# One program block for attention, its general path and the expert layers; the first tokens prepared inside the last pair of heads; alpha transposed behind all of y

## The reference

```python
# attention: q, k, v, alpha are (4, 8, 768, 48), alpha in 0.8 to 1.0
for t in range(S):
    state = alpha[:, :, t, :, None] * state + k[:, :, t] (x) v[:, :, t]
    y[:, :, t] = q[:, :, t] @ state
x = y as 3072 tokens x 384                      # transpose and reshape
# first layer, d_ff 2048
h = x @ w_in
g = (a0 + a1*h + a2*h^2 + a3*h^3) / (1 + |b0||h| + |b1|h^2 + 1e-6)
x2 = g @ w_out
# second layer, d_ff 1024
h = x2 @ w_in2;  solu = h * softmax(h)
out = layernorm(solu) * g_ln @ w_out2
```

## Time and profile before

| | us |
|---|---|
| median of 3 runs | 836.74 (834.29 to 837.64) |
| profiled execution, its own time | 835.56 |
| span of its instructions | 833.8 |
| busy: PE, PEld | 787.8, 733.2 |
| busy: DVE, ACT, POOL | 689.5, 606.4, 313.1 |
| mean granted TensorE clock | 0.987 |

### The profile page before, as it was taken

How to read it: one execution, slowest core, us unless ns; L and a number is a source line. 1 busy time by engine, 2 the same in 40 slices (tenths; PEclk the granted TensorE clock), 3 DMA queues, 4 the chain that set the end, 5 groups by cost and what they waited for, 6 DMA issues and landing times.

```text
span 833.8 us, 16287 instructions
## 1 busy us (share of the span) xinstructions
PE 787.8 (94%) x5378; PEld 733.2 (88%) x5378; DVE 689.5 (83%) x1248; ACT 606.4 (73%) x1258; POOL 313.1 (38%) x376
## 2 busy tenths in 40 slices
PE   5989999869889999999999999999999999999986
PEld 4777777769879999999999999999999999999975
DVE  5888888669999888988889888898889888898642
ACT  5777788568878776887678867787778777687522
POOL 5999886412223222332223323232333322233201
PEclk8999999999999999999999999999999999999998
DMA  8999997410000010001000100000000000000000
GB/s 178 223 233 234 241 206 180 110 44 1 19 11 1 11 39 1 11 11 39 9 1 9 38 9 0 12 36 9 9 28 9 9 9 9 1 11 10 11 9 29
DMA packets 113174, 42.96 MB, mean 52 GB/s; under 512 B 101616, under 2 KB 110960, under 8 KB 113136
## 3 DMA queue, kind: packets, MB, share of 16 engines
q1 hardware_dynamic: 110336, 33.04, 16.8%
q0 software_dynamic: 2800, 9.45, 3.9%
HBM read 33.04 MB, written 9.44 MB: 51 GB/s over the span
## 4 chain that ended last, share of the span: by engine, by line
PE 61%; DVE 10%; ACT 6%; issue 2%; DVEq 0%; POOL 0%; ACTq 0%
PE h_ps L919 17%; PE acc_ps L945 17%; PE y_ps L901 13%; PE z_ps L964 12%; DVE work L1160 2%; PE z_ps L974 2%; DVE rec L1152 2%; DVE den L1148 2%; ACT rec L1054 1%; ACT g_hi L1044 1%; DVE den L1165 1%; ACT rec L1056 1%; DVE solu L1124 1%; DVE work L1168 1%; ACT den L1019 1%
## 5 line engine op out<-in xcount | busy, mean ns | idle before, releaser
L1102 POOL TENSOR_TENSOR g_lo<-work,g_hi 128x384 fp32r<-128x384 f32 x128 | 130.8, 1022 | 406.0 <-ACT g_hi L1044 406.0
L919 PE MATMUL h_ps<-x,w 128*128 (+1 forms) x1152 | 227.8, 342 | 9.8 <-DVE work L1170 4.6
L945 PE MATMUL acc_ps<-g_hi,w 128*128 128x384 f32 x768 | 218.4, 338 | 2.2 <-POOL g_lo L1102 2.2
L919 PEld LDWEIGHTS h_ps<-x,w 128*128 128x128 f32 x1152 | 203.5, 189 | 16.0 <-DVE work L1170 8.8
L945 PEld LDWEIGHTS acc_ps<-g_hi,w 128*128 128x128 f32 x768 | 141.2, 188 | 2.8 <-POOL g_lo L1102 2.8
L1016 ACT ACTIVATE h<-h_ps 128x384 f32<-128x384 f32 x128 | 61.7, 482 | 101.9 <-PE h_ps L919 101.9
L945 PE MATMUL acc_ps<-g_lo,w 128*128 128x384 f32 x384 | 129.6, 338 | 0.0
L901 PE MATMUL y_ps<-w,lnT 128*128 128x384 f32 x576 | 111.8, 344 | 2.7 <-DVE ysb L1191 2.7
L1165 DVE SCALAR_TENSOR_TENSOR den<-h,ncoef,den 128x384 f32<-128x384 f32 x128 | 78.6, 614 | 42.5 <-ACT den L1019 41.5
L901 PEld LDWEIGHTS y_ps<-w,lnT 128*128 128x128 f32 x576 | 104.8, 193 | 4.9 <-DVE lnT L1182 3.0
L964 PE MATMUL z_ps<-w,x 128*128 128x512 f32 x414 | 104.3, 397 | 3.3 <-DVE lnT L1182 3.3
(11 more groups left out here) (116 smaller groups left out, 1140.8 us busy)
## 6 DMA issues: line engine op xcount, KB each, us to landing
work<-in_alpha_dram SPq DMA_DIRECT2D x32, 144.0 KB, 3.4
chunks_xin<-in_q_dram SPq DMA_DIRECT2D x32, 144.0 KB, 3.2
chunks_xin<-in_k_dram SPq DMA_DIRECT2D x32, 144.0 KB, 3.1
chunks_vin<-in_v_dram SPq DMA_DIRECT2D x16, 288.0 KB, 4.0
wstage<-in_moe_w_in_dram POOLq DMA_DIRECT2D x9, 512.0 KB, 4.8
attention_out<-solu SPq DMA_DIRECT2D x32, 144.0 KB, 3.1
out_dram<-ysb SPq DMA_DIRECT2D x24, 192.0 KB, 1.8
x<-attention_out SPq DMA_DIRECT2D x7, 576.0 KB, 3.9
```

The costliest lines, as they stand in the source:

```text
L919: mm = nc.tensor.matmul(h_ps[s % 2][:, 0:TT], w1[:, wz, kc, s * P:(s + 1) * P], xs[:, xz, kc, :], start=(n == 0), stop=(n == 3 * KC - 1))
L945: mm = nc.tensor.matmul(acc_ps[:, dc, 0:TT], w2[:, wz, f, dc * P:(dc + 1) * P], rhs, start=(f == 0 and n == 0), stop=(f == FC1 - 1 and n = ...
L1102: nc.gpsimd.tensor_tensor(g_lo[:, 1 - o, :], gate[:, 1 - o, :], g_hi[:, 1 - o, :].bitcast(F32), ALU.subtract).then_inc(glo_done, 1)
```

## The change

It has four parts.

1. The three blocks become one. `attention_by_chunks` and `attention_by_scan` now return their programs for each engine, and these are called at the head of the layers' block. The barriers go. In their place the four engines with a branch wait for a semaphore `judged`, which comes with `fits`; POOL, PE and DVE then raise `joined`, and every engine waits for `joined` = 3 and for all 32 y copies before its part of the layers.
2. In body 16 (the last pair's stage 2) ACT makes the high part of the first tokens at the head of the body, DVE the low part ahead of its first mask, and PE the first chunk of h between turning kp back and the products of chunks 4 and 5. It waits there for all weight pieces. For this the tile `x` takes the place of tiles that are dead by then, and `h_ps` is the tile that was `turn_aq`. The general path makes the three again from its own results.
3. The transposes of alpha stand behind `before` of chunks 3 to 5, in every body.
4. In body 16 the counting matmul stands ahead of that last `before`.

```diff
+def first_h(nc, over):
+    KC, TT = over.x.shape[3:]
+    for kc in range(KC):
+        for n, (wz, xz) in enumerate(PARTS):
+            mm = nc.tensor.matmul(over.h_ps[:, 0, 0:TT], over.w1[:, wz, kc, 0:P], over.x[:, 0, xz, kc, :],
+                                  start=(kc == 0 and n == 0), stop=(kc == KC - 1 and n == 2))
+    return mm
...
 # attention_by_chunks, tensor, body
                         mm.then_inc(kt_turned, 1)
+            if i_is(n, NPAIR):
+                pe.wait_ge(w_lo, over.w_pieces)
+                pe.wait_ge(over.x_ready, over.x.shape[3])
+                first_h(nc, over).then_inc(over.h_ready, 1)
...
                         for c in range(CPH + 1, NC):
                             within(p, c)
+                if i_is(n, NPAIR):
+                    pe.wait_ge(tally, 6)
+                    nc.tensor.matmul(ring[0:1, 0, 0:1], okay[:, 4:5], ones[:], start=True, stop=True).then_inc(counted, 1)
+                for c in range(CPH, NC):
+                    mm = before(p, c)
+                mm.then_inc(y_done, 1)
                     if stage1(n + 1):
                         pe.wait_ge(a_loaded[1 - o], (i + o + 1) * 32)
                         pe.wait_ge(rec_done, n + 1)
                         turn(ain[:, 1 - o], turn_aq, a_turned, CPH)
-                    if stage2(n):
-                        for c in range(CPH, NC):
-                            mm = before(p, c)
-                        mm.then_inc(y_done, 1)
...
 # scalar, body
+            if i_is(n, NPAIR):
+                act.wait_ge(x0_loaded, 16)
+                act.wait_ge(k_turned, NPAIR)
+                act.wait_ge(ksq_seen, NPAIR)
+                for kc in range(over.x.shape[3]):
+                    nc.scalar.activation(over.x[:, 0, HI, kc, :], x0_of(over.work, *over.x.shape[3:])[:, kc, :],
+                                         ACT.Copy).then_inc(over.xhi_done, 1)
...
 # vector, body
+            if i_is(n, NPAIR):
+                dve.wait_ge(kp_ready, NPAIR)
+                for kc in range(over.x.shape[3]):
+                    dve.wait_ge(over.xhi_done, kc + 1)
+                    nc.vector.tensor_tensor(over.x[:, 0, LO, kc, :], x0_of(over.work, *over.x.shape[3:])[:, kc, :],
+                                            over.x[:, 0, HI, kc, :].bitcast(F32), ALU.subtract).then_inc(over.x_ready, 1)
...
 # attention_by_scan, tensor (gpsimd, sync and vector alike)
-            @block.tensor
-            def _(pe):
+    def tensor(pe):
+        pe.wait_ge(judged, 1)
                 with pe.If(pe.value_load(fits, min_val=0, max_val=1) != 1):
...
+        pe.sem_inc(joined, 1)
...
 # the layers' block
+        def attention_over(eng):
+            eng.wait_ge(joined, 3)
+            eng.wait_ge(att_copied, NB * NH)
...
             def _(pe):
+                chunks.tensor(pe)
+                scan.tensor(pe)
+                attention_over(pe)
...
-                        if g is not None:
+                        if g is not None and not (i_is(i, 0) and s == 0):
...
             def _(act):
+                chunks.scalar(act)
+                attention_over(act)
...
-                for kc in range(KC):
-                    x_hi(0, kc)
...
-                for kc in range(KC):
-                    x_lo(0, kc)
```

More of the change, by code:

```diff
@@ L39 @@
 PARTS = ((HI, HI), (HI, LO), (LO, HI))
+@dataclass
+class Programs:
+    sync: object
+    gpsimd: object
+    tensor: object
+    scalar: object
+    vector: object
+@dataclass
+class Handover:
+    work: object
+    x: object
+    w1: object
+    h_ps: object
+    att_stored: object
+    x0_loaded: object
+    xhi_done: object
+    x_ready: object
+    h_ready: object
+    y_copied: object
+    judged: object
+    w_pieces: int
 def wait_alone(eng, semaphore, value, carrier):
@@ L172, in halves @@
             return t.rearrange("p (z t) -> p z t", z=2)
[L174 to L246, removed]
-            @block.tensor
-            def _(pe):
[L250 to L255, removed]
-                def attention_products(p, chunks):
-                    for c in chunks:
-                        for j in range(2):
-                            rows = slice(j * HB, j * HB + D)
-                            mm = nc.tensor.matmul(ring[:, j, (c % 4) * P:(c % 4 + 1) * P], kp[rows, c * P:(c + 1) * P],
-                                                  qp[rows, p, c * P:(c + 1) * P], start=True, stop=True)
-                    mm.then_inc(att_done, 1)
-                def within(p, c):
@@ L478, in attention_by_scan @@
+    return Programs(sync, gpsimd, tensor, scalar, vector)
+def attention_by_scan(nc, ctx, q, k, v, alpha, scratch, ident, fits, w_lo, neg_done, solu, over):
     NB, NH, S, D = q.shape
@@ new lines, in gpsimd @@
+    def gpsimd(pool):
+        pool.wait_ge(judged, 1)
+        with pool.If(pool.value_load(fits, min_val=0, max_val=1) != 1):
+            pool.wait_ge(y_copied, NB * NH)
+            nc.gpsimd.memset(xin[:], 0.0).then_inc(zeroed, 1)
+            nc.gpsimd.memset(blockones[:], 0.0).then_inc(zeroed, 1)
+            pool.wait_ge(zeroed, 2)
+            for j in range(2):
+                nc.gpsimd.memset(blockones[j * HB:(j + 1) * HB, j * HB:(j + 1) * HB], 1.0).then_inc(zeroed, 1)
+                pool.wait_ge(zeroed, 3 + j)
+            nc.gpsimd.tensor_tensor(onehot[:], ident[:, 0:HB], ident[:, HB:P], ALU.add).then_inc(zeroed, 1)
+            pool.wait_ge(zeroed, 5)
+        pool.wait_ge(w_lo, over.w_pieces)
+        pool.wait_ge(neg_done, 1)
+        pool.sem_inc(joined, 1)
@@ L658, in build @@
         solu = sb("solu", [P, F2])
+        h_ps = ps("h_ps", [P, 2, 512])
+        with ExitStack() as guests:
+            homes = [sb("chunks_" + name, shape, F32, guests) for name, shape in
+                     (("xin", [P, 2, S // P, HB + D]), ("rec", [P, S]), ("err", [P, S]), ("att", [P, 2, S // P, P]), ("causal", [P, P]), ("okay", [P, 5]))]
+        x = sb("x", [P, 2, 2, KC, TT], F32R)
         phase_a = ExitStack()
```

723 lines of the change are left out of this document (401 added, 322 removed).

## The result

| | before | changed |
|---|---|---|
| median, us | 837.19 (834.29 to 837.96, 4 runs) | 827.08 (825.71 to 828.42, 4 runs) |
| profiled execution, its span | 835.56, 833.8 | 826.95, 825.2 |
| mean granted clock | 0.987 | 0.996 |

The ratio is 0.9885 (95%: 0.9856 to 0.9915): 10 us faster, where 827.5 was forecast. Two later sets of runs of the same kernel gave 0.9919 (0.9889 to 0.9949) and 0.9883 (0.9857 to 0.9909), so the gain is 7 to 10 us.

The account below looks back on a forecast made before the run. It took a ring of waits among ACT, DVE and TensorE to bound the attention, and the layers' start to bound the rest. 3.9 + 4.7 + 0.7 - 0.3 = 9.0 us gave 827.5 us, range 824 to 831.

Parts of the forecast that it names:

- last `kp` to first square, clock apart: From the last pair to the layers: ACT's first h at K+12.85 instead of K+17.53, 4.7 us gained (K: last `kp` start).
- second h late: In the layers: the second chunk's h, due in 2.73 us, takes 3.3 at the lower clock; 0.3 us charged.
- the ring through ACT's copy, `err` and `rec`: In each attention pair: ACT, DVE and TensorE wait on one another in turn, said to set the 9.50 us period.
- the ring that the prediction named: In each pair after the change: scans, mask, TensorE's work up to alpha, alpha's transposes, scans; 9.2 us.
- The period: Attention, scans to scans of two pairs: 9.2 us instead of 9.50, 3.9 us over 13 periods.
- The rival of the transfers: Attention: transfers keep the period at 9.5 us, only the handover's 5.1 us is gained, 831.6 us; chance 0.12.
- The start: First pairs of the attention: the first alpha moved behind `before` costs about 0.7 us.
- Splits and h inside the last pair: Last pair: nine matmuls of h from K+3.6 in 1.6 us, products of chunks 4 and 5 from K+5.2.
- The handover: Attention to layers: reading `fits` and the branch stay, 1.35 us, starting only once `before` has left TensorE's queue.
- The clock: Last pair and handover: fewer TensorE pauses keep 0.7 us of clock; 0.3 us is charged for the second h.
- ACT's wait for `before` gone: Attention: a sign of being right, with a wait for the transposes of kp in its place.
- The slower rival: Attention: 14 pairs pay 0.85 us for late alpha, 11.9 against 5.1 from the handover, 843.5 us; chance 0.05.

Follow-up runs that it names:

- The filler: Four idle matmuls per pair ahead of alpha's transposes: in the changed kernel, behind `before`, 837.95 us; in the changed kernel with part 3 undone, 834.02 us.
- these six profiles: Three profiles of the changed kernel and three with the store of y put ahead of v's load (826.59 us; with 26 idle matmuls too, 824.35 and 825.38 us).
- alpha in front: The changed kernel with part 3 undone, alpha's transposes ahead of the last `before`: 831.5 us, ratio 0.9934 to the kernel before.
- part 3 alone: The kernel before with only alpha's transposes moved behind the last `before`, three blocks as they were: 832.28 us, ratio 0.9952.
- the change without part 2: The changed kernel with the split and first h put back at the head of the layers, still one block: 830.63 us, ratio 0.9932.
- three blocks: The changed kernel with part 1 undone, three blocks with their barriers, the rest of the change kept: 830.49 us, ratio 0.9930.
- 26 matmuls ahead: The changed kernel with 26 idle identity matmuls in TensorE's pauses before the second pair: 825.45 us, ratio 0.9877; also run with the earlier store.

## Why the prediction was right

The forecast was 9.0 us less for the profiled execution; the span fell by 8.6. The terms, each read from the two profiled runs:

| term | forecast | measured |
|---|---|---|
| 13 periods | 3.9 | 123.53 - 119.10 = 4.4 |
| third pair's scans later | -0.7 | 24.81 - 27.85 = -3.0 |
| last scans to last `kp` | 0.7 | 8.46 - 7.71 = 0.75 |
| last `kp` to first square, clock apart | 4.7 | 5.2 |
| clock kept in the last products | 0.7 | 6.07 + 0.2 - 5.03 = 1.2 |
| second h late | -0.3 | 0 |
| sum | 9.0 | 8.6 |

- **Which ring binds.** Right. Taking out the ring through ACT's copy, `err` and `rec` left the ring that the prediction named. The filler shows it: 0.94 us longer behind y, 0.2 in front.
- **The period.** The mechanism was right; 9.2 was 9.06. The pieces were 1.91 instead of 1.98 up to the mask, 5.57 instead of 5.68 to the end of `within`, 0.15 instead of 0.09, 0.58 instead of 0.60. In the profiled run the disturbed pairs took back 1.3 us of that.
- **The rival of the transfers.** Wrong as a period, since it fell to 9.06, but its ground was there: late transfers cost 0 to 3.2 us in these six profiles. I had held against it that no engine waits for a load. That was so before, but the earlier trace rows has only three of the waits, and the full list has ACT waiting for a store, 1.6 us in 3 waits. With the shorter period that became 6.0 in 4, and TensorE waited for q's load in several runs, up to 1.7 us at a time. The queues moved nearly the same before and after (237 and 239 GB/s), so no run shows whether they would carry a yet shorter period.
- **The start.** The term that was mis-sized most: 0.7 us for the first alpha behind `before`, measured 3.0. The sum had no term for the clock at the start. Behind 13.2 us the lower level held for some 11.7 us instead of 6.8, through work that is the same in both. Other profiles separate this from the order. Where k's six loads at 20.5 to 21.0 us had the full clock's length (0.62 or 0.63), the third scans came at 24.95, 25.17 and 25.39 with alpha behind, and at 25.37 with alpha in front and the filler; where those at 21.5 to 21.9 had it, without the filler, they came at 25.95 to 26.27; and where those at 22.2 us still had the lower clock's length, at 27.85, and at 27.31 with alpha in front. So the surplus goes with the clock of the run and not with the order. The order's own share, 24.95 to 25.39 against 24.81 before, is 0.1 to 0.6 us, at or below the forecast, though the clock's course is not quite the same in these runs. Why the level lasts longer in one run than in another stays open.
- **Splits and h inside the last pair.** Right: nine matmuls of h from K+3.51 in 1.53 us (K+3.6 and 1.6 forecast), the last products at K+5.30 (K+5.2).
- **The handover.** Right in kind, too dear by 0.6 us. The step that failed: "it can only start when `before` is out of TensorE's queue". TensorE's queue in the changed kernel (names, then ns, then start), to be held against the earlier trace rows:

```profile
L621 PEldq TENSOR_LOAD <-fits x1: 491/491/491, 164.3 to 164.3; - x1
...
L621 PEldq COMPARE_BRANCH  x1: 356/356/356, 165.2 to 165.2; - x1
```

  The flag is read at 164.3, right behind `fits` (164.15 to 164.29), while `before` still runs until 164.94. Reading and branch cost the same 1.2 us or so as before, but 0.6 of it lies beside the matmuls. The jump itself took 0.36 us, not more than the 0.37 before, so no added stall showed. From the end of `before` to ACT's first square it is 0.77 us, not 1.4.
- **The clock.** It was undervalued. Kept were 1.2 us in the products and the 0.3 charged to the second h. But I laid the fall ahead of 160.8 to pauses such as the 0.88 us, and credited the matmuls of h with the cure. With part 3 alone and with the change without part 2, both without those matmuls, the same pause of 0.88 us stands there and the clock stays full (4.91 and 5.03 us from products to copy); without part 3, but with the matmuls, it stays full too (165.85 to 170.89). So that pause by itself does not bring the clock down. The kernel before has one profile only, and whether its low clock there is a matter of its order or of that run stays open, and with it the 1.2 us. At the handover the runs agree: TensorE's pauses of 4.63 us (before), 4.65 (part 3 alone), 3.99 (three blocks) and 2.31 (without part 2) were followed by the lower level, those of 1.0 to 1.2 us in the others were not.
- **The signs.** "ACT's wait for `before` gone" was wrong: 10.7 us remain, 0.84 a pair. It no longer costs anything, since ACT catches up before `ktok`. The last `kp` came at 154.66, not 153.
- **The slower rival.** DVE does wait 0.4 us for alpha in each pair, but that wait stands in a shorter ring; nothing is lost.

By ratios, against the mean of the changed kernel's three (0.9896), the parts are worth 3.2 us (part 3), 3.0 (part 2) and 2.8 (part 1), each with some 2 us of uncertainty. Part 4 was not tried by itself. That 827.08 and 827.5 are so near is partly luck: two misses of the attention (+0.5, -2.3) and one of the handover (+1.4) nearly cancel.

## What to carry to other kernels

When a pause of one engine ends a ring, add up the next ring from the same timeline before changing the order; it told the new period to 0.14 us. A filler on the engine in question, in the old order and in the new, shows in two runs which ring binds. Work that is ready early is best put ahead of the last dependent piece, where it also shortens the pause at the handover, behind which the clock fell here; and one profile holds a late transfer or a clock level that the next one doesn't, so judge terms of one or two us by several.

## What the runs showed of the hardware

- Three blocks with two barriers, and the issue of the last stores and a branch between them, left ACT idle for 3.17 us; with semaphores in one block it was 0.23. The reading of a flag began while earlier matmuls of the same engine ran (164.3 against 164.94).
- All profiles without matmuls ahead start at the lower clock (six loads in 1.11 us at 7.65 us). In some it was full at 13.2 to 13.6 us and low again for 6.8 us; in others it was still low there, in one run until about 24.9. The profile's granted clock shows 1.00 there until its first recorded fall. With 26 matmuls ahead two of three runs had the lower level again behind a later wait of 1.77 and 1.91 us; the third, which waited 1.25 us there, did not.
- A DMA share of 1.00 is no wall for the period: a pair went from 9.50 to 9.06 us with the share at 1.00 to 1.01. Beside it stood single late stores and loads, up to 3.8 us, whose number differs from run to run; at a share of 0.94 they were nearly gone.
- Four idle float32 matmuls of 128 by 128 showed as eight weight loads, 0.97 us.
